# SyncE issues the copies of q into its stacks before the fetch of the reciprocal rows, in a thresholded-attention kernel on one Trainium2 core

## The reference

```python
scores = scale * np.matmul(q, k.transpose(0, 1, 3, 2))
thresh = np.max(scores, axis=-1, keepdims=True) - tau
scores = np.where(scores >= thresh, scores, -1000000000.0)
attn = np.exp(scores - np.max(scores, axis=-1, keepdims=True))
attn = attn / (np.sum(attn, axis=-1, keepdims=True) + 1e-09)
out = np.matmul(attn, v)
```

## Time and profile before

| | |
|---|---|
| median of 3 runs | 1299.22 us (1296.48 to 1300.75) |
| the profiled execution, its own time | 1297.2 us |
| its span, first to last instruction | 1295.4 us |
| outside the span | 1.8 us |
| granted TensorE clock, mean | 0.997 |
| attention, all 32 pairs | about the first 573 us |

### The profile page before, as it was taken

The page is one execution under the profiler, slowest core; times in us unless marked ns, Lnnn a source line. Parts: engine busy times, 40 slices in busy tenths (PEclk is TensorE's granted clock), DMA queues, the critical chain, the costliest instruction groups (busy, mean ns, idle before and its releaser), DMA issues.

```text
span 1295.4 us, 29432 instructions
## 1 busy us (share of the span) xinstructions
PE 1266.9 (98%) x9396; PEld 1138.1 (88%) x9396; DVE 924.1 (71%) x2153; ACT 797.9 (62%) x1727; POOL 336.6 (26%) x372
## 2 busy tenths in 40 slices
PE   7999999999999999999999999999999999999999
PEld 6777777777777777779999999999999999999998
DVE  4888888888888888868676666657655766566554
ACT  4878888888888888865544454455445544544432
POOL 2465556666655565443000000000000000000000
PEclk8999999999999999999999999999999999999999
DMA  6456666666666665412001101110110011001001
GB/s 150 108 148 154 166 155 160 157 151 151 149 159 167 157 168 140 124 39 88 18 19 36 35 9 37 36 36 1 36 44 26 12 36 35 17 28 36 17 1 42
DMA packets 136824, 105.12 MB, mean 81 GB/s; under 512 B 91424, under 2 KB 108064, under 8 KB 136736
## 3 DMA queue, kind: packets, MB, share of 16 engines
q1 hardware_dynamic: 135232, 103.40, 30.8%
q10 hardware_dynamic: 1504, 0.62, 0.2%
HBM read 54.56 MB, written 19.02 MB: 57 GB/s over the span
## 4 chain that ended last, share of the span: by engine, by line
PE 71%; SPq 12%; DMA 9%; ACT 3%; issue 3%; DVE 1%; ACTq 0%; DVEq 0%
PE score_ps L974 31%; PE score_ps L1061 16%; DMA q_all<-q_lo 9%; PE aux_ps L1045 8%; PE aux_ps L582 6%; PE aux_ps L498 5%; PE score_ps L540 5%; SPq L345 5%; ACT probs L627 2%; SPq L336 2%; SPq L303 2%; SPq L338 1%; SPq L304 1%; SPq L286 1%; ACT recip_T L610 0%
## 5 line engine op out<-in xcount | busy, mean ns | idle before, releaser
L540 PE MATMUL score_ps<-k_all,q_all 128*128 128x288 f32 x1280 | 241.8, 316 | 18.8 <-DMA q_all<-q_lo 12.5
L707 DVE SCALAR_TENSOR_TENSOR probs<-score_ps,threshold,probs 128x576 f32<-128x576 f32 x288 | 230.5, 817 | 36.2 <-ACT probs L627 31.4
L695 DVE TENSOR_REDUCE neg_max<-score_ps 128x1 f32<-128x576 f32 x288 | 217.4, 756 | 50.7 <-PE score_ps L540 50.5
L974 PE MATMUL score_ps<-xm_hi,w_lo 128*128 128x288 f32 x768 | 225.9, 294 | 1.7 <-ACT r_tanh L1158 1.7
L974 PE MATMUL score_ps<-xm_hi,w_hi 128*128 128x288 f32 x768 | 226.5, 295 | 0.0
L974 PE MATMUL score_ps<-xm_lo,w_hi 128*128 128x288 f32 x768 | 226.4, 295 | 0.0
L627 ACT ACTIVATE probs<-score_ps,neg_max 128x576 f32<-128x576 f32 x288 | 208.1, 737 | 16.2 <-DVE neg_max L695 11.2
L540 PEld LDWEIGHTS score_ps<-k_all,q_all 128*128 128x128 f32 x1280 | 180.6, 191 | 29.3 <-DVE probs L707 26.7
L498 PE MATMUL aux_ps<-ident,probs 128*128 128x128 f32 x1280 | 191.1, 276 | 1.1 <-ACT probsT_rem L610 0.6
L610 ACT ACTIVATE probsT<-aux_ps 128x512 f32<-128x512 f32 x288 | 166.9, 591 | 25.9 <-PE aux_ps L498 18.2
L498 PEld LDWEIGHTS aux_ps<-ident,probs 128*128 128x128 f32 x1280 | 147.9, 140 | 30.2 <-issue 27.5
(11 more groups left out here) (90 smaller groups left out, 2316.7 us busy)
## 6 DMA issues: line engine op xcount, KB each, us to landing
k_all<-k_all SPq DMA_DIRECT2D x31, 320.0 KB, 4.4
q_all<-q_lo SPq DMA_DIRECT2D x62, 160.0 KB, 3.6
recip_rows<-recip_scratch SPq DMA_DIRECT2D x64, 144.0 KB, 4.4
x_scratch<-x_out SPq DMA_DIRECT2D x32, 288.0 KB, 2.1
out<-y SPq DMA_DIRECT2D x36, 256.0 KB, 2.0
k_all<-k_all SPq DMA_DIRECT2D x31, 288.0 KB, 3.5
v_nat<-in_v SPq DMA_DIRECT2D x32, 256.0 KB, 2.8
qk_nat<-in_q SPq DMA_DIRECT2D x63, 128.0 KB, 2.6
```

The lines of the kernel that those rows point to most:

```text
L540: last = nc.tensor.matmul(ps[:, half, 0:HALF], query(h, i, par), kk[par][:, at:at + HALF], start=(n == 0), stop=(n == len(terms) - 1))
L695: nc.vector.tensor_reduce(neg_max[:, turn, 0:1], scored(i), mybir.AxisListType.XY, ALU.max, negate=True).then_inc(max_ready, 1)
L707: nc.vector.scalar_tensor_tensor(tile_halves(i), scored(i), threshold[:, turn:turn + 1], tile_halves(i), ALU.is_ge, ALU.mult, accum_out=ro ...
L974: last = nc.tensor.matmul(ps, w, m, start=(n == 0), stop=(n == 3 * len(terms) - 1))
```

## The change

In SyncE's run, `stack_q` of the next pair now stands ahead of `fetch_rows` of the pair before. Nothing else differs, and the transfers themselves are the same.

```diff
                 if c < PAIRS - 1:
                     stack_k(it, c + 1)
+                if c < PAIRS - 1:
+                    stack_q(sp, it, c + 1)
                 if c > 0:
                     fetch_rows(it, c - 1)
-                if c < PAIRS - 1:
-                    stack_q(sp, it, c + 1)
                 if weight:
                     load_w(it, c, *weight)
```

## The result

The changed kernel takes 1279.93 us in the median of 4 runs (1279.07 to 1281.41), against 1299.15 before: a ratio of 0.9855, 95% interval 0.9836 to 0.9874. The forecast was 1282, in a range of 1278.5 to 1289. The profiled executions took 1297.2 and 1280.31 us, 16.9 less, and their spans 1295.4 and 1278.4, 17.0 less.

The account below looks back on a forecast made before the run. PE was taken as the bound, 98% busy, standing still 19.3 us for q's landing at 30 seams; less 30 x 0.08 for a new stall, 16.9 us off the median 1299.22 gave 1282, range 1278.5 to 1289.

Parts of the forecast that it names:

- 30 seams: PE's passages to the next pair's first score tile, runs 1 to 30; line 540's loads stood still 19.3 us there.
- The wait charged to a mask of DVE: PE's loads at the seam: the profile named DVE's mask as releaser; the prediction disbelieved it, mask over 0.37 us before.
- Step 1: SyncE's queue: q's copies go out at about 269.4 in place of 270.84, a lead of 1.44 us.
- Step 2: DMA: q lands earlier, by 1.44 us by issue or 1.25 to 1.4 by bytes, and is no longer last.
- Step 3: PE at each seam: a new stall of 0.08 us behind ACT's copy of rem0; the seam gives 0.56 of 0.63.
- Step 4: Whole kernel: 19.3 - 30 x 0.08 = 16.9 us won, bounds 12.3 and 19.3; a run takes 16.7 us.
- Step 5: GpSimd's normalize and SyncE: rows land later, at about 275.1, costed at nothing because the cover holds, barely.
- The rule that the prediction weighed: DMA engines take descriptors in ring order, so q no longer waits for the rows' writes and the rows wait for q's.
- SyncE's ring: Fetch, landing, normalize, store, loads, send, copies, fetch: 16.4 us; rows landing in 5.0 leave half the gain, 1291; chance 0.09.
- the slower rival: The same ring through SyncE outlasts the old 17.3 us run if rows take over 5.4 us to land; chance 0.04.
- q's landing isn't what holds: PE's seam: DVE's mask holds the loads, so no change, 1299 us; shares chance 0.05 with q's landing not moving.
- PE has room all over: PE's whole run: it could shrink by q's full lead of 1.4 us, 42 us in all, to 1257; chance 0.02.

Follow-up runs that it names:

- the second profile of before: The kernel before, unedited, run once more with a profile: 1295.9 us.
- double_fetch: The changed kernel with each fetch of rows issued twice, the second into a tile nobody reads, all behind q's copies: 1319.28 us, ratio 1.0175.
- rows_after_v: The changed kernel with both fetches of rows moved further back, behind the loads of v: 1342.43 us, ratio 1.0337.
- one_head: The kernel before with one 288 KB transfer of the first head's reciprocals to 128 partitions in place of two of 144 KB: 1315.7 us, ratio 1.0134.

## Why the prediction held, step by step

**What bounded it.** Right. The 19.3 us at 30 seams were q's landing, and all but 0.4 went. The wait charged to a mask of DVE vanished too when only q and the rows changed places, and scores3 now starts before that mask is over, so the name was wrong and the length right.

**Step 1, the issue.** Right: q goes out behind q_lo at once (0.03 us) in the run shown and in nearly all. In four runs of the loop SyncE comes to it late, so that the second copy goes out 0.9 to 1.4 us after q_lo and not 0.55. In each of these four, two small loads for the mixing stages stand ahead of the loads of q and k in its queue. The latest is the run behind which PE still waits, the 0.4 us that are left in its row. Its second copy took 0.88 in place of 0.60, part of the full queue that I had bounded.

**Step 2, the landing.** Right in size: 1.5 us earlier, against 1.25 to 1.44 forecast. The runs went further, and split the 1.5 in two. With the issues left and the bytes gone the landing moved by 1.0 us. The changed kernel differs from that run in that q's second copy goes out 1.55 us earlier after q_lo, and this brought the landing forward by only 0.45 more. So, counted in this order, two thirds of what the change gives q comes from taking 288 KB from ahead of it in the DMA engines. What the 2.06 us in SyncE's queue cost by themselves, with the rows' bytes still ahead, no run shows.

**Step 3, what is late next.** Right: ACT's copy of rem0, at 0.10 us in one run of two where I said 0.08. In the other run, at the loop's turn, scores3 starts some 0.1 late (a run of 16.8 and not 16.66), which I hadn't forecast and haven't explained.

**Step 4, the sum.** 16.9 forecast, 16.9 measured between the profiled executions. That it fits to a tenth is luck: the seams of the second profile of before hold 1.6 us less, and the medians differ by 18.0 to 19.2. Where the 1 to 2 us above the sum lie is open. A run of 16.7 was forecast, 16.73 measured.

**Step 5, the rows.** Right: they land some 0.35 us after PE's scores3, normalize waits for them for 0.9 us (x_raw is there at 248.98, it starts at 249.92), and GpSimd still idles 2.17 us before its next work. The rule that the prediction weighed fits: q's and the rows' landings keep the order of issue in every row shown, and the rows landed 3.55 us after their second issue, not 4.4. SyncE's wait for recip_T shrank, from 77.9 us in 31 waits to 41.6 in 21 over the kernel.

**The rivals.** SyncE's ring is real, and by the estimate above the changed kernel stands a few tenths of a microsecond from it. In the changed kernel a late SyncE holds PE up once, for 0.4 us; two more issues turn the gain into a loss of 1.75%, which is the slower rival at work. That q's landing isn't what holds was refuted by the order of before with the rows' bytes gone, where q lands earlier and the seam's wait is gone. That PE has room all over was refuted by the run, which became 0.6 us shorter where q's landing moved by 1.5: the rest of q's lead was not there to be won.

## What to carry to other kernels

Ask of each transfer on a critical queue who waits for it, and put last what has cover: here the order alone was worth 1.4%, and the bytes that stood ahead of q were by themselves enough to make PE wait. Then follow the ring that the moved transfer now lies in (landing, its reader, the next thing behind it on the same queue) and sum it up against the new, shorter period; the cover of before counts less than it looks, since every engine's period shrinks with the gain. An upper bound on such a gain is what the engine stands still there, and the next wait behind it can be read from the same timeline: look for the operation that ends within a few tenths of where the first would be.

## What the runs showed of the hardware that I had not expected

- The time of a DMA's issue depends here on its place behind others more than on itself. The fourth issue, counted from k's first copy, is the long one, whatever it is: the second fetch of rows 1.27 us in the kernel before, q's second copy 1.27 in double_fetch and rows_after_v, q's first copy 1.24 in one_head and 1.20 with one fetch ahead. Cutting a fetch from 144 KB to 2 KB left its issue as long. With the pause for q_lo it is 0.88. The count holds for this series alone: counted from send_recip, whose two issues go straight ahead, the fourth is k's second copy, at 0.61 to 0.63.
- One transfer of 288 KB to 128 partitions from one row of DRAM took 6.1 us to land, two of 144 KB to 64 each from a row of its own 4.4. The same bytes with an outer dimension of 2 used a tenth of the engines' time, as two of the sixteen would, and cost 195 us over the kernel.
